# Pairs of heads packed into nine key chunks, the low part of g moved to VectorE, other score pieces, and the second expert matrix as the stationary operand, in a fused attention and two-layer expert kernel

## The reference

```python
scores = q @ k^T / sqrt(D)                      # 2 x 8 heads, 576 x 576
kth    = 32nd largest of each row
attn   = softmax(where(scores >= kth, scores, -1e9))
x      = (attn @ v) as rows                     # 1152 x 512
h      = x @ w_in                               # 1152 x 2048
y      = (h * cos(h)) @ w_out                   # 1152 x 512
expert = argmax(y @ w_gate), weight = softmax at it       # 8 experts, capacity 288
out[i] = weight[i] * relu(y[i] @ w1[e]) @ w2[e]           # w1: 512 x 1024, w2: 1024 x 512
```

## Time and profile before

| what | value |
|---|---|
| median of 3 runs | 710.23 us (707.17 to 712.25) |
| profiled execution, its own time | 708.68 us |
| its span, first to last instruction | 706.9 us |
| mean granted TensorE clock | 0.980 |
| busy: TensorE (PE), its weight loads (PEld) | 640.7, 553.2 us |
| busy: VectorE (DVE), ScalarE (ACT), GpSimd (POOL) | 497.2, 434.2, 324.2 us |
| DMA | 68.61 MB, 97 GB/s over the span |

### The profile page before, as it was taken

The page is one execution under the profiler, slowest core; times in us unless marked ns, Lnnn a source line. Parts: engine busy times, 40 slices in busy tenths (PEclk is TensorE's granted clock), DMA queues, the critical chain, the costliest instruction groups (busy, mean ns, idle before and its releaser), DMA issues.

```text
span 706.9 us, 12925 instructions
## 1 busy us (share of the span) xinstructions
PE 640.7 (91%) x4210; PEld 553.2 (78%) x4210; DVE 497.2 (70%) x953; ACT 434.2 (61%) x675; POOL 324.2 (46%) x326
## 2 busy tenths in 40 slices
PE   5678698799999999999999998989978999999996
PEld 3466497598797797887987987988867888888884
DVE  5991999995894984994994975011725678776673
ACT  2654666658758668678677686662726455566550
POOL 0364657558557567487386485671410111011111
PEclk9999999899999999999999999999989999999999
DMA  5963700000000000000000000014159456675510
GB/s 168 375 259 121 290 9 5 1 28 5 15 13 5 24 5 5 23 5 5 22 4 4 15 0 0 17 31 194 74 195 352 148 196 258 262 278 218 191 46 15
DMA packets 17791, 68.61 MB, mean 97 GB/s; under 512 B 1998, under 2 KB 6606, under 8 KB 15056
## 3 DMA queue, kind: packets, MB, share of 16 engines
q1 hardware_dynamic: 16000, 63.27, 23.5%
q0 software_dynamic: 1744, 4.73, 2.0%
HBM read 54.33 MB, written 14.45 MB: 97 GB/s over the span
## 4 chain that ended last, share of the span: by engine, by line
PE 66%; ACT 12%; POOL 9%; issue 7%; DMA 3%; DVE 2%; POOLq 0%; ACTq 0%; SPq 0%; DVEq 0%
PE p_o L1161 8%; PE p_a L1198 7%; PE p_s L1125 6%; PE p_t L1141 5%; PE p_b L1198 4%; PE p_b L1220 4%; PE p_b L1222 3%; PE p_b L1221 3%; POOL h_sb L648 3%; ACT L845 2%; PE p_s L1361 2%; PE p_t L1361 2%; PE p_o L1378 2%; POOL g_lo L654 2%; PE p_o L1379 2%
## 5 line engine op out<-in xcount | busy, mean ns | idle before, releaser
L362 DVE MAX8 top<-arena 128x8 f32<-128x576 f32 x288 | 201.3, 747 | 16.8 <-ACT arena L796 16.8
L365 DVE MATCH_REPLACE8 arena<-top,arena 128x576 f32<-128x576 f32 x216 | 158.9, 744 | 0.0
L615 POOL TENSOR_TENSOR arena<-arena,pen 128x576 f32<-128x576 f32 x72 | 100.7, 1416 | 63.9 <-ACT pen L803 63.9
L1161 PEld LDWEIGHTS p_o<-arena,probsT 128*128 128x128 f32 x640 | 88.2, 213 | 23.0 <-ACT probsT L821 15.5
L1161 PE MATMUL p_o<-arena,probsT 128*128 128x65 f32 x640 | 90.5, 294 | 13.2 <-ACT probsT L821 11.5
L372 DVE TENSOR_SCALAR den<-o_sb 128x8 f32<-128x8 f32 x9 | 4.7, 517 | 103.8 <-ACT o_sb L827 103.8
L1220 PE MATMUL p_b<-w_out_lo,g_hi 128*128 128x512 f32 x144 | 64.0, 444 | 14.5 <-POOL g_lo L654 13.8
L821 ACT COPY probsT<-p_t 128x640 f32<-128x640 f32 x72 | 50.0, 695 | 42.2 <-PE p_t L1141 42.1
L1125 PE MATMUL p_s<-arena,q_sb 64*128 64x224 f32 (+5 forms) x320 | 64.2, 510 | 8.4 <-DMA arena<-in_kt 4.3
L1141 PE MATMUL p_t<-ident,arena 128*128 128x128 f32 x360 | 56.4, 292 | 15.2 <-ACT arena L814 15.2
L1198 PE MATMUL p_a<-xT,wff 128*128 128x128 f32 x512 | 65.2, 281 | 0.0
(11 more groups left out here) (171 smaller groups left out, 1288.4 us busy)
## 6 DMA issues: line engine op xcount, KB each, us to landing
arena<-in_w SPq DMA_DIRECT2D x8, 2048.0 KB, 9.0
wff<-in_w SPq DMA_DIRECT2D x8, 2048.0 KB, 9.3
slot_rows<-y_now SPq DMA_DIRECT2D x1, 4626.0 KB, 14.6
wff<-in_w_out SPq DMA_DIRECT2D x1, 4096.0 KB, 12.1
wff<-in_w_in SPq DMA_DIRECT2D x1, 4096.0 KB, 22.0
wff<-slot_rows SPq DMA_DIRECT2D x8, 385.5 KB, 3.7
arena<-in_vones SPq DMA_DIRECT2D x2, 1300.0 KB, 16.6
q_sb<-in_q SPq DMA_DIRECT2D x36, 64.0 KB, 2.5
```

What stands on the lines that cost most here:

```text
L362: nc.vector.max(best, src).then_inc(top_step, 1)
L365: nc.vector.match_replace(work[:, a, :], best, src, LOWEST).then_inc(top_step, 1)
L615: nc.gpsimd.tensor_tensor(s_sb[:, t, :], s_sb[:, t, :], pen[:, t % 2, :], ALU.subtract).then_inc(masked, 1)
L1161: last = mm(p_o[:, col:col + VC], probsT[:, P * c:P * c + P], vones[batch][:, c, t, :], start=(c == 0), stop=(c == NVC - 1))
```

## The change

1. **Nine chunks for a pair.** The exponentials of two heads stand side by side (1152 columns = 9 x 128), so chunk 4 holds the end of one head and the start of the next. Chunks are turned and copied three at a time (group g = 0 to 11 in a block) into two halves of `probsT`. `vones` is packed to match; chunk 4 is multiplied with 130 columns. The exponential of the next pair's first head waits until group 1 of this pair is turned, that of its second head until group 2 is.
2. **The low part of g** is made by VectorE, between `pair_top` calls: pieces 0 and 1 after pair 1, pieces 2 and 3 after pair 2. GpSimd's `masks` and `bias` move in its order, and so do ScalarE's `pens`, `cosines`, `high_g` and `copy_o`. In body 1 `reciprocals` stand one pair later; in body 0 the exponentials stand ahead of `high_w_out`, and `keep_warm` adds two float32 products of 512 columns after each pair.
3. **Score pieces** are 160, 416, 416 and 160 keys.
4. **Experts.** w2 is stationary: the second layer is two units of two output chunks, 64 products as in the first layer, with sums by ScalarE and VectorE and eight back-turns (`turn_back`). `w1_hi` and `w2_hi` have two homes, and their rounding is spread over the expert before. `keep` copies weights and row numbers out of `rows` on VectorE, two small copies for each expert.

The core of the diff:

```diff
-SPOT = [288 + 512, 512 - 288]
-SPLIT = [512 - 288, 288]
+SHORT = 160
+SPOT = [512 - (S - SHORT), 1024 - SHORT]
...
+                if down:
+                    low_g(i - 2, 0)
+                    low_g(i - 2, 1)
                 pair_top(i, 2)
                 if down:
+                    low_g(i - 2, 2)
+                    low_g(i - 2, 3)
                     reciprocals(i - 1)
                 pair_top(i, 3)
...
-                for c in range(NVC):
-                    k = P * c if c < NVC - 1 else LAST
-                    last = nc.tensor.transpose(p_t[:, P * c:P * c + P], probs[:, t % 2, k:k + P], ident[:])
+                for c in range(GROUP):
+                    k, at = P * (GROUP * (g % 3) + c), 512 * (g % 2) + P * c
+                    last = nc.tensor.transpose(p_t[:, at:at + P], probs[:, k:k + P], ident[:])
...
+                for p in range(H // 2):
+                    g = 3 * p
+                    transpose_probs(i, g)
+                    if not up:
+                        transpose_probs(i, g + 1)
+                    if more:
+                        scores(i + 1, p, next_keys)
+                    if p == 3 and down:
+                        gate(i - 2)
+                    part(2 * p, 0)
+                    if up:
+                        transpose_probs(i, g + 1)
+                    times_v(i, g, mixed, batch)
+                    part(2 * p, 1)
+                    transpose_probs(i, g + 2)
...
+                    times_v(i, g + 1, mixed, batch)
+                    part(2 * p + 1, 0)
...
+                    times_v(i, g + 2, mixed, batch)
+                    part(2 * p + 1, 1)
+                    if not up:
+                        keep_warm()
...
+                copy_pT(i, 9)
+                if more:
+                    pens(i + 1, 0)
+                cosines(i - 1, 1)
+                copy_pT(i, 10)
+                if more:
+                    scores(i + 1, 3)
+                copy_pT(i, 11)
                 if more:
                     exp_tile(i + 1, 0)
-                    scores(i + 1, 3)
-                    pens(i + 1, 1)
+                high_g(i - 1, 2)
...
+                            if f < FC2 - 1:
+                                mm(bank_d[:, 0:2 * m], w2_hi[j][:, f, cols], both_he, start=(f == 0), stop=False)
+                                mm(bank_d[:, 0:m], w2_lo[j][:, f, cols], high_he, start=False, stop=False)
```

More of the change, by code:

```diff
@@ L478, in _ @@
             last = NBLK - 1
+            low_g(last - 1, 0)
+            low_g(last - 1, 1)
             reciprocals(last)
@@ L494, in gated, with low_w1 @@
                 nc.vector.tensor_tensor(h_sb[:, part], h_sb[:, part], turns[:, part], ALU.mult).then_inc(g_ready, 1)
[L496 to L503, removed]
+            def low_w1(E, j, pieces=range(4)):
+                for c in pieces:
                     wait(dve, w1_hi_made, 4 * E + c + 1)
@@ L514, in _ @@
             place_first()
-            low_g(0)
-            low_g(1)
+            low_g(last, 0)
+            low_g(last, 1)
             fraction(2)
@@ L649, in gated @@
                                         ALU.mult).then_inc(g_ready, 1)
-            def low_g(i, c):
-                wait(pool, g_hi_made, 4 * i + c + 1)
-                part = slice(512 * c, 512 * c + 512)
-                nc.gpsimd.tensor_tensor(g_lo[:, part], h_sb[:, part], g_hi[:, part].bitcast(F32),
-                                        ALU.subtract).then_inc(g_lo_made, 1)
             def low_w_out(c):
@@ L1094, in expert @@
+                copy_cross(E, 1, n)
+                high_he(E, 0, n)
+                if begin:
+                    high_w2(E, j, turn, 0)
+                elif more:
+                    high_w1(*after, (1,))
+                copy_cross(E, 2, n)
+                high_he(E, 1, n)
+                if begin:
+                    high_w2(E, j, turn, 1)
+                copy_cross(E, 3, n)
+                high_he(E, 2, n)
+                if begin:
+                    high_w2(E, j, turn, 2)
                 high_he(E, 3, n)
+                if begin:
+                    high_w2(E, j, turn, 3)
@@ L1095, in expert @@
                 if more:
                     high_x(E + 1, n)
-                    high_w1(E + 1, 1 - j, turn + j)
+                    high_w1(*after, range(4) if begin else (2, 3))
+                    high_w2(*after, 0)
+                copy_cross(E, 4, n)
+                if more:
+                    for c in range(1, 4):
+                        high_w2(*after, c)
+                if not more:
+                    copy_cross(E, 5, n)
             high_x(0, ROUNDS[0][1])
@@ L1384, in _ @@
+                turn_back(E, 0, n)
+                if not more:
+                    turn_back(E, 1, n)
             turn_rows(0, 0, 0, ROUNDS[0][1])
```

421 lines of the change are left out of this document (243 added, 178 removed).

## The result

The changed kernel takes **689.3 us** (684.15 to 690.4, four runs) against 710.5 beside it on the same chip: a ratio of 0.9692, interval 0.9641 to 0.9743. The forecast was 674 with a range of 658 to 691: the sign and the range held, but of the 36 us only 21 came.

A forecast was written before the change was run, and what follows sets the result against it. TensorE was taken to bound the loops and experts, VectorE the run-up. Gains of 21.6 (loops), 11 (run-up), 2 (end of attention) and 1 (experts) sum to 35.6 us off 708.68: 673.1, as a median 674 us; range 658 to 691.

The forecast's parts named there:

- the experts' term: Experts: 0.4 us gained in each of seven, 1 in the first, 3 lost at the end: 1 us gained.
- rival (a): Loops: VectorE becomes the bound through the lock or late `g_hi`; block stays at 48.6 us, time 688; chance 0.16.
- the end of attention: Last block and the wait for its x: 2 us gained in all (0 to 4).
- Rival (c): Experts: they lose 8 us, since VectorE's order holds the sums that free TensorE's banks; time 684; chance 0.10.
- The loops: Six blocks: each goes from 50.0 to 46.4 us (45.2 to 48.6), 21.6 us gained.
- scores of a pair: Loops, TensorE: new score pieces cut a pair from 1.44 to 1.16 us, 1.1 us for a block.
- Waits for `g_lo`: Loops, TensorE: about 1 us of waiting stays in a block (0 to 2.5), where 1.5 or more was.
- the wait that I had put at `copy_pT(10)`: Loops: this copy stands behind a sine that waits for GpSimd's `fraction`; 0.5 us of new waiting a block (0 to 1.5).
- the loop that I drew through the search of pair 2: Loops, VectorE: reciprocals, `g_hi`, `low_g`, pair 2, next reciprocals; caps the block at 48.6 us unless `g_hi` comes earlier.
- A `low_g` beside GpSimd: Loops, VectorE: takes 0.70 us or longer; by the lock rule it would wait for 0.4 on average.
- The run-up: Before the loops: a search fills VectorE's idle 15.06 us and body 1 shortens; 11 us gained (4 to 16).
- Rival (b): Run-up: body 0 stays at TensorE's half rate, so the run-up gives 4 us; time 682; chance 0.12.

The follow-up runs named there:

- experiment 1: The changed kernel with `keep` moved behind everything else VectorE does for an expert: 664.65 us, ratio 0.9389.
- experiment 5: The changed kernel, `keep` in its early place, with SyncE holding the load of w1 until the sends of the expert before are done: 664.8 us, ratio 0.9388.
- the staircase: Block times: 50.05 us in the kernel before, 49.18 with nine chunks and new orders, 48.66 with the new pieces, 46.28 with `low_g` on VectorE.
- Experiment 9: The kernel before with only the four g_lo of a block moved to VectorE, ScalarE's and GpSimd's orders kept: 707.28 us, ratio 0.9963.
- experiment 7: The kernel of experiment 1 with g_lo of the loops back on GpSimd: 687.05 us, ratio 0.9693.
- Experiment 10: The kernel of experiment 1 with body 1's reciprocals after pair 0, as in the kernel before, not after pair 1: 671.07 us, ratio 0.9455.
- experiment 3: The changed kernel with the old score pieces of 224, 352 and 288 keys: 692.25 us, ratio 0.9782.
- experiment 8: The kernel before with only the new score pieces of 160 and 416 keys: 705.55 us, ratio 0.9964.
- experiment 11: The kernel of experiment 1 with body 0's exponentials behind the two casts of w_out again, as in the kernel before: 668.13 us, ratio 0.9433.

## Why the prediction was right in sign and 15 us short

**The failed step is the experts' term**, "7 x 0.4 + 1 - 3 = 1 us gained (from 8 lost to 6 gained)". It measured 15.8 lost, outside its own bounds. The two small copies of `keep` were counted as work ("gets two more sums and two small copies", covered by VectorE's free time in 14.9 us an expert), and the wait that they bring was not looked at: `keep` overwrites row numbers that a send two experts back still reads, so VectorE has to wait for a DMA in the middle of its order. And the sends were counted only at the end of the kernel ("both scalings and sends follow in a row"): that they come 7.4 us later inside each expert, where the load of w1 is issued 0.16 us behind them, was not looked at, and there a send takes 8.18 us instead of 2.9. Neither half costs anything alone: experiment 1 leaves the collision and takes the wait out of the way, experiment 5 leaves the wait and takes the collision away, and both give 664.7. Without it the experts take 177.3 from the first turn of rows, 2.6 less than before, against the 1 forecast, a difference within what this stretch varies between traces; the steps are 20.4 where I said 20.8.

That 689.3 lies in the range is in part luck: the upper end of 691 was set for rival (a), which did not come, and 3.7 us more than forecast from the end of attention made up for some of the loss.

Rival (c) named the right place, VectorE's order, and half of the loss; its reason, sums that free TensorE's banks, was only the last link of the chain.

**The loops** held: 46.26 for a block against 46.4. The terms: scores of a pair 1.17 for 1.16; the copy of 384 columns 0.481 for 0.48; three turns 0.33 and six products of v 0.62, as counted. TensorE's waits are 0.6 us in a block against the 1.5 I left in it (0.4 for a copy of probabilities, 0.2 for x), and its own work is 45.3 for the 44.9 that I summed. Waits for `g_lo` are gone, where I left 1 us. So two small errors of opposite sign met. What I had wrong is where the part comes from: I drew the gain of a block from TensorE's saved work, 2.3 of 3.6, and the move of `g_lo` as a cost to be bounded. By the staircase the chunks with the new orders, which no run separates, give 0.87, the pieces 0.52 and the move 2.4, since it takes 2.5 us out of the way from `g_hi` over GpSimd's `fraction` to ScalarE's sine, and with it the wait that I had put at `copy_pT(10)`.

**Rival (a)** did not come. Experiment 9, with the old order of ScalarE, has a late `g_hi` and a block of 49.4, but not by the loop that I drew through the search of pair 2: VectorE is idle for 3.90 us behind that search, so `g_hi` is late by itself. What I said against the rival, "3 us of ScalarE work leave the way of g_hi", fits the two blocks, but no run moves ScalarE's order alone. A `low_g` beside GpSimd was foretold at 0.70 or longer and is 0.811 in the mean of the block, 0.97 at 118.67, where GpSimd's `gated` is at work for 0.42 more. The Trainium skill (SBUF — State Buffer, "SBUF: two separate sides") names an exclusive lock, and by my estimate from it a `low_g` would wait for 0.4 on average; the rows have 0.11 more than the 0.70 of the earlier trace rows. The trace agrees with the rule all the same, and my estimate was at fault, since it took the meetings to be at random. Of the four `low_g` of the middle block, those at 350.50 and 351.11 meet no GpSimd instruction and take 0.69 and 0.68; those at 338.13 and 338.84 start when GpSimd has 0.24 and 0.55 left, and take 0.78 and 1.09, so each ends 0.54 after GpSimd. In the same way `den` takes 0.96 where it meets GpSimd's `g_lo` in experiment 7 and 0.17 in the changed kernel.

**The run-up**, 11.8 for 11. Experiment 10 shows its main part, the search in VectorE's hole (8.6 with what the clock adds), and experiments 3, 7 and 8 show that the pieces (3 to 4) and the move (6) have shares too, so the parts overlap. The exponentials have 3 us by experiment 11, but not by shortening a step of body 0, as I had it. Rival (b) did not come: from 65 to 77 us TensorE does still run at half rate for a part (six products of v 1.54 at 67.53 against 0.62), but it has time there, and without `keep_warm` the time is the same.

**The end of attention**: I count six blocks as 6 x 3.79 = 22.7, which leaves 28.4 - 22.7 = 5.7 for the last bodies against 2 (0 to 4). The wait of TensorE for x of the last block, 1.97 in the earlier trace rows, is 0.19. What of the other 2 to 3 us is the clock and what the earlier `low_g` was not taken apart; this stays open.

**The sum**: 22.7 + 11.8 + 5.7 + 0.1 - 15.8 = 24.5, forecast 35.6. With the experts at 2.6 gained instead, it is 43 us, and experiment 1 has 708.7 - 665.0 = 43.7 in the profiled executions.

## What to carry to other kernels

Count the waits of a new small instruction, not its length: a copy of 0.15 us in the middle of an engine's order cost 3.6 to 5.2 us each time, since it waited for a DMA and everything behind it on the engine waited too; put such copies behind the work that feeds the bound engine. When a change moves a transfer, look at what else is issued at its new time. And judge the parts of a change together: the same move of work was worth 0.7 us a block in the old kernel and 2.4 in the new one.

## What the hardware showed that I had not expected

A send by GpSimd's queue of 96 rows lands in 2.9 us (the median of the kernel before) and takes 8.2 to 9.1 when a load of 2 MB is issued 0.16 to 0.22 us behind it, and holding the load back for 3.5 us costs nothing that shows (664.8 against 664.65). TensorE's clock is a second price of a stall: behind a wait of 6.09 us the next products start 0.43 apart for some 5 us, behind one of 1.60 they start 0.23 apart; the kernel in which TensorE arrives earlier at the same wait is 3.5 us slower (668.13 against 664.65), of which the clock's share is argued and not measured alone. In two experts of the changed kernel (545 to 594 us) a form of 384 columns has a mean of 435 ns that is 360 ns long in experiment 1. And a `low_g` on VectorE that starts while a GpSimd instruction is at work ends about 0.55 us after it (GpSimd has 0.24 left: 0.78; 0.55 left: 1.09; in experiment 9 1.03 left: 1.58), where it takes 0.69 alone.
